# First quarter of a linear-attention kernel: alpha, key and query fetched as three-token runs, and another order of the first weight pieces

## The chip, the cores and the metric

The kernel runs on one core of one Trainium2 chip. The metric is the device time of one launch in microseconds (us), the median of three runs.

## The reference, cut to what matters

Three stages follow each other: a gated linear attention (a state of 48 by 48 for each head, decayed by alpha at each token), a SiLU-gated feed-forward layer behind an RMS norm, and a second layer with four experts that are weighted by domain probabilities.

```python
for t in range(S):                       # B=2, H=8, S=768, D=48
    state = alpha[:, :, t, :, None] * state + einsum('bhd,bhe->bhde', k[:, :, t], v[:, :, t])
    y[:, :, t] = einsum('bhd,bhde->bhe', q[:, :, t], state)
x = y.transpose(0, 2, 1, 3).reshape(1536, 384)
xn = x / sqrt(mean(x * x) + 1e-6) * rms_g
x = (silu(xn @ w_gate) * (xn @ w_val)) @ w_out          # 384 -> 1536 -> 384
out = sum over e of p[:, e] * (relu(x @ w1[e]) @ w2[e]) # 4 experts, 384 -> 1024 -> 384
```

## The kernel before, in words

The 1536 tokens are cut into four quarters of 384, a quarter into three chunks of 128. Within a quarter the eight heads are taken in four pairs. For one pair the alpha, key and query rows are transposed on TensorE (`T`, `TK`, `TQ`), VectorE makes the running product of alpha (a scan over a chunk) and scaled keys and queries (`M`), TensorE makes scores and a key-value sum (`S`, `KV`), VectorE masks the scores (`S`) and carries the state (`ST`), and TensorE adds up the output (`Y`). The first quarter's steps stand in a list written out by hand, `FIRST`; the later quarters' attention steps are placed between the matmuls of the first feed-forward layer by the generator `events()`. Every engine runs its own instructions of that one order, and semaphores tie them together.

`a_tm`, `k_tm` and `q_tm` hold a quarter token by token: partition p holds token p of each chunk, and a head takes 64 columns, 48 of data and 16 that were set to one. `load_quarter` fills them with one DMA per chunk, in rows of 48 floats (192 bytes). The first quarter is loaded in two halves of four heads; the last four heads come first, because pair 3 goes first. Alpha is clamped in place by VectorE (step `C`). All of alpha is also loaded a second time (`alpha_all`, eight parts) and tested on ScalarE for values outside the range (steps `E 0` to `E 7`).

The weights of the first layer are cut into twelve pieces, gate, val and out for each of four column groups. A piece goes into one of two staging slots (`load_piece(n)` waits in front of its DMA until piece n-2 has been split), and POOL splits it into a high and a low part: one `TENSOR_SCALAR` over 1152 elements, then three `TENSOR_TENSOR` over 384 (`split`). The semaphore `s_wlo` counts finished splits. POOL splits the first `EARLY` pieces ahead of everything else, and then one piece per step `V` of the first quarter. In step `V 0` the pieces of work on POOL are: `hidden_lo(0)`, the high part of the next piece, `hidden_lo(1)`, the low part. `hidden_lo(n)` is what TensorE needs for its matmuls of step `O n`. The first matmuls of this layer, `G 0` and `V 0`, need pieces gate 0 and val 0, `O 0` to `O 2` need out 0, `G 3` and `V 3` need gate 1 and val 1.

All loads are issued by SyncE (SP), one after another. A wait in front of one DMA holds all behind it. `fill_holes(0)` is six small DMAs of that queue: they bring the rows of the last head pair from `x_last` into the gaps of `x_raw`, and the norm, and so the first feed-forward matmul, waits for the last of them. `next_a(1)`, `next_kq(1)` and `next_v(1)` load the second quarter, three DMAs for each of alpha, key, query and value. TensorE needs its query rows in the transposes (`TQ`) just ahead of `O 0`.

```python
def load_piece(n):
    m, g = PIECES[n]
    slot = n % 2
    if n >= 2:
        sp.wait_ge(s_wlo, n - 1)
        sp.wait_ge(s_whi, n - 1)
...
if i == 0 and f < NPIECE - EARLY:
    split(pool, EARLY + f, None if f else lambda: hidden_lo(1))
```

Of the kernel before, what the change touches and what calls it, by code (L numbers as in the profile page):

```python
# [12 lines left out]
P = 128  # L13
LANE = 64
CH = 128
NCH = 3
# [10 lines left out]
def gated_attention_two_moe(nc, q, k, v, alpha, w_gate, w_val, w_out, rms_g, probs, w1, w2, out):  # L27
# [16 lines left out]
    with ctx:  # L44
        def sem(name):
            return ctx.enter_context(nc.semaphore(name))
# [81 lines left out]
        wvh = sb("wvh", [P, KT, FF], F32R, reg_b)  # L128
        wvl = sb("wvl", [P, KT, FF], F32R, reg_b)
        woh = sb("woh", [P, FT, DM], F32R, reg_b)  # L130
        reg_w = ExitStack()
# [108 lines left out]
        s_half = [sem(f"s_half{i}") for i in range(4)]  # L240
        s_clamp = sem("s_clamp")
        s_w = [sem("s_w0"), sem("s_w1")]
# [113 lines left out]
        PW = FF // NQ  # L356
        PIECES = [(m, g) for g in range(NQ) for m in ("gate", "val", "out")]
        EARLY = 3
        HI = {"gate": wgh, "val": wvh, "out": woh}
# [31 lines left out]
        for place in AT.values():  # L391
# [8 lines left out]
        FIRST = [(name, int(f)) for name, f in  # L400
                 (step.split() for step in ("F 10", "C 0", "T 0", "T 1", "TK 0", "TQ 0", "TK 1", "TQ 1", "F 5", "M 0",
# [45 lines left out]
        def _(sp):  # L447
            def load_quarter(i, which, first_head=0, last_head=H, arrived=None):
                b, t0 = i // QB, (i % QB) * TQ
                hs = slice(first_head, last_head)  # L450
                src, dst, done = ((alpha, a_tm, s_qka[0]), (k, k_tm, s_qka[1]), (q, q_tm, s_qka[2]), (v, v_tm, s_v))[which]
                for c in range(NCH):
                    sp.dma_start(dst[:, c, :].rearrange("p (h x) -> p h x", h=H)[:, hs, 0:D],  # L453
                                 src[b, hs, t0 + c * CH:t0 + (c + 1) * CH, :].rearrange("h p d -> p h d")
                                 ).then_inc(arrived or done, 16)
# [45 lines left out]
            for which in (0, 1, 2):  # L501
                load_quarter(0, which, 0, H // 2)
                if which == 0:
                    load_alphas(0)
            load_alphas(1)
            load_alphas(2)
            load_quarter(0, 3, 0, H // 2)
            load_alphas(3)
# [6 lines left out]
            rows_to_lanes(sp, gcol[:, :].rearrange("p (j n) -> p j n", n=1), rms_g.rearrange("(r n) -> r n", n=1),  # L515
                          s_small, True)
            fill_holes(0)
            next_a(1)
            load_piece(2)
            next_kq(1)  # L520
            sp.dma_start(prob[:, :, :], probs.rearrange("(t p) e -> p t e", p=P)).then_inc(s_prob, 16)
            load_piece(3)
            sp.wait_ge(s_wild, 1)
# [83 lines left out]
        def _(pool):  # L607
# [42 lines left out]
            assert made[0] == CONST_ALL  # L650

            for n in range(EARLY):
                split(pool, n)
# [105 lines left out]
        def _(act):  # L759
# [11 lines left out]
            def squares(j, done=s_sq):  # L771
                act.activation(x_nrm[:, j, :], x_raw[:, j, :], ACT.Square).then_inc(done, 1)

            for name, i, f in events():
                u = NP * i + f
# [186 lines left out]
        def _(dve):  # L962
# [59 lines left out]
            for name, i, f in events():  # L1022
                u = NP * i + f
                if name == "C":

                    part = a_tm[:, :, :]
                    if i == 0:
                        part = a_tm[:, :, 0:H // 2 * LANE] if f else a_tm[:, :, H // 2 * LANE:]
                    if i == 0 and f == 0:
                        dve.wait_ge(s_half[0], 16 * NCH)  # L1030
                    else:
                        dve.wait_ge(s_qka[0], 16 * NCH * (i + 1))
                    dve.tensor_scalar(part, part, MID - HALF, MID + HALF, ALU.max, ALU.min).then_inc(s_clamp, 1)
                elif name == "T":
# [294 lines left out]
        def _(pe):  # L1329
# [21 lines left out]
            for name, i, f in events():  # L1351
# [11 lines left out]
                if name in ("T", "TK", "TQ", "AHEAD"):  # L1363
# [3 lines left out]
                    for which, tm, bank, done in todo:  # L1367
                        if which and i == 0 and f < 2:
                            pe.wait_ge(s_half[which], 16 * NCH)
                        elif which:  # L1370
                            pe.wait_ge(s_qka[which], 16 * NCH * (i + 1))
                        else:

                            pe.wait_ge(s_clamp, 1 if i == 0 and f < 2 else i + 2)
                            if i and f == 0:
                                pe.wait_ge(s_rinv, i)
                            wait_two(pe, s_sm, i, f, 2)
                        if which == 1:
                            wait_two(pe, s_st, i, f, NCH)
                        if which == 2 and i:  # L1380
                            pe.wait_ge(s_wild, 1)
                            wait_three(pe, s_yc, i, f, 2)
                        for c in range(NCH):
                            mm = pe.transpose(banks[bank][:, c * CH:(c + 1) * CH],  # L1384
                                              tm[:, c, n * 2 * LANE:(n + 1) * 2 * LANE], ident[:, :])
                        mm.then_inc(done, 1)
# [247 lines left out]
```

## Time and profile before

| | us |
|---|---|
| median of three runs | 700.92 |
| lowest and highest | 700.06 and 701.42 |
| the profiled execution's own time | 701.39 |
| its span on the chip | 699.3 |
| TensorE busy | 685.6 |
| VectorE, ScalarE, POOL busy | 460.1, 260.1, 320.1 |

The span runs from the first to the last instruction; what lies around it is 2.1 us. TensorE is busy for 98% of the span. The times in the rows further down are counted from the span's start.

### The profile page before, as it was taken

The numbers are of one execution on the slowest core, as the hardware profiler recorded it, in microseconds if no ns is written. First come the engines' busy times: TensorE is split into PE (matmuls) and PEld (weight loads), VectorE is DVE, ScalarE is ACT, GpSimd is POOL, SyncE is SP. The second block draws the span as 40 slices with busy tenths as digits, with TensorE's granted clock in tenths as the row PEclk, the third lists the DMA queues.
The fourth block names the chain that finished last, engine by engine and source line by source line (L and its number), as shares of the span: only waits on it lengthen the run. The fifth ranks groups of instructions, "written<-read, shape, count | busy, mean of one in ns | idle before, by whom it ended". The sixth has DMA issues, their size and how long they took to land.

```text
span 699.3 us, 10687 instructions
## 1 busy us (share of the span) xinstructions
PE 685.6 (98%) x3998; PEld 635.2 (91%) x3998; DVE 460.1 (66%) x808; ACT 260.1 (37%) x472; POOL 320.1 (46%) x401
## 2 busy tenths in 40 slices
PE   7799999999999999999999999999999999999998
PEld 6689999999999999998899999999999999999997
DVE  6875666655556543306848777877797778777875
ACT  4831334222522243227314343434343334433430
POOL 3469761121111114740394585458645764577200
PEclk9999999999999999999999999999999999999999
DMA  8994480005102000100001101110011101100003
GB/s 183 207 198 112 102 171 0 9 1 103 35 1 77 1 2 27 65 0 1 1 22 47 46 5 42 46 46 22 24 46 46 38 9 46 45 24 1 23 0 136
DMA packets 71748, 35.13 MB, mean 50 GB/s; under 512 B 53904, under 2 KB 70672, under 8 KB 71696
## 3 DMA queue, kind: packets, MB, share of 16 engines
q1 hardware_dynamic: 71696, 34.44, 19.7%
q8 instruction: 32, 0.52, 0.3%
q14 instruction: 20, 0.16, 0.1%
HBM read 31.48 MB, written 2.36 MB: 48 GB/s over the span
## 4 chain that ended last, share of the span: by engine, by line
PE 89%; SPq 6%; DVE 2%; issue 1%; DMA 1%; POOL 1%; ACT 0%; DVEq 0%
PE out_ps L1341 13%; PE out_ps L1343 13%; PE out_ps L1342 13%; PE hid_ps L1334 7%; PE hid_ps L1336 7%; PE hid_ps L1335 7%; PE at_ps L1546 4%; PE at_ps L1545 4%; PE at_ps L1544 4%; SPq L453 4%; PE hid_ps L1545 2%; PE hid_ps L1546 2%; PE hid_ps L1544 2%; PE at_ps L1384 2%; SPq L444 1%; PE at_ps L1398 1%
## 5 line engine op out<-in xcount | busy, mean ns | idle before, releaser
L1216 DVE SCALAR_TENSOR_TENSOR x<-out_ps,prob,x 128x384 f32<-128x384 f32 x180 | 110.4, 613 | 58.7 <-PE out_ps L1343 58.7
L1341 PE MATMUL out_ps<-early_r,late_r 128*128 128x384 f32 x384 | 129.1, 336 | 0.3 <-DVE x L1216 0.3
L1342 PE MATMUL out_ps<-early_r,late_r 128*128 128x384 f32 x384 | 129.4, 337 | 0.0
L1343 PE MATMUL out_ps<-early_r,late_r 128*128 128x384 f32 x384 | 129.3, 337 | 0.0
L671 POOL TENSOR_TENSOR hid_lo<-act_sb,hid_hi 128x384 fp32r<-128x384 f32 x44 | 44.9, 1020 | 167.6 <-ACT hid_hi L859 167.6
L915 ACT COPY late<-at_ps 128x512 f32<-128x512 f32 x98 | 57.7, 589 | 108.0 <-PE at_ps L1546 105.1
L1181 DVE TENSOR_TENSOR act_sb<-hid_ps,act_sb 128x384 f32<-128x384 f32 x48 | 26.6, 555 | 80.2 <-PE hid_ps L1336 70.9
L1341 PEld LDWEIGHTS out_ps<-early_r,late_r 128*128 128x128 f32 x384 | 72.1, 188 | 6.6 <-DVE x L1216 0.9
L1342 PEld LDWEIGHTS out_ps<-early_r,late_r 128*128 128x128 f32 x384 | 72.0, 188 | 5.3
L1343 PEld LDWEIGHTS out_ps<-early_r,late_r 128*128 128x128 f32 x384 | 72.1, 188 | 0.0
L725 POOL TENSOR_TENSOR early<-stage 128x128 f32<-128x128 f32 x14 | 6.5, 465 | 129.6 <-PE at_ps L1546 102.6
L859 ACT CAST hid_hi<-act_sb 128x384 fp32r<-128x384 f32 x48 | 24.6, 513 | 107.9 <-DVE act_sb L1181 107.9
L1341 PE MATMUL out_ps<-hid_hi,woh 128*128 128x384 f32 x144 | 50.8, 352 | 0.6 <-DVE hid_lo L1185 0.6
L1334 PE MATMUL hid_ps<-xn_hi,wvh 128*128 128x384 f32 x141 | 49.3, 349 | 0.8 <-POOL wvl L603 0.7
L1546 PE MATMUL at_ps<-late_r,early_r 128*128 128x512 f32 x126 | 50.0, 397 | 0.0
L1334 PE MATMUL hid_ps<-xn_hi,wgh 128*128 128x384 f32 x141 | 49.2, 349 | 0.2 <-DVE act_sb L1168 0.2
L1269 DVE TENSOR_TENSOR at_ps<-at_ps,late 128x512 f32<-128x512 f32 x70 | 48.7, 695 | 0.5
L1544 PE MATMUL at_ps<-late_r,early_r 128*128 128x512 f32 x126 | 48.9, 388 | 0.0
L1343 PE MATMUL out_ps<-hid_hi,wol 128*128 128x384 f32 x144 | 48.3, 335 | 0.0
L1342 PE MATMUL out_ps<-hid_lo,woh 128*128 128x384 f32 x144 | 48.2, 335 | 0.0
L1336 PE MATMUL hid_ps<-xn_hi,wvl 128*128 128x384 f32 x141 | 47.3, 335 | 0.0
L1335 PE MATMUL hid_ps<-xn_lo,wvh 128*128 128x384 f32 x141 | 47.2, 335 | 0.0
(272 smaller groups left out, 1613.7 us busy)
## 6 DMA issues: line engine op xcount, KB each, us to landing
stage<-in_moe_w_dram SPq DMA_DIRECT2D x32, 384.0 KB, 3.4
alpha_all<-in_alpha_dram SPq DMA_DIRECT2D x8, 288.0 KB, 6.8
stage<-in_moe_w_out_dram SPq DMA_DIRECT2D x4, 576.0 KB, 4.1
out_dram<-x SPq DMA_DIRECT2D x12, 192.0 KB, 1.9
stage<-in_moe_w_gate_dram SPq DMA_DIRECT2D x8, 216.0 KB, 4.0
stage<-in_moe_w_val_dram SPq DMA_DIRECT2D x8, 216.0 KB, 4.1
a_tm<-in_alpha_dram SPq DMA_DIRECT2D x9, 192.0 KB, 4.1
k_tm<-in_k_dram SPq DMA_DIRECT2D x9, 192.0 KB, 4.4
```

The source lines that it names most:

```text
L671: pool.tensor_tensor(hid_lo[:, n % 2, :], act_sb[:, n % 2, :], hid_hi[:, n % 2, :].bitcast(F32), ALU.subtract).then_inc(s_hl, 1)
L915: act.copy(tcp[n], bank).then_inc(s_copy, 1)
L1216: dve.scalar_tensor_tensor(out=a, in0=part, scalar=p, in1=a, op0=ALU.mult, op1=ALU.add).then_inc(s_acc, 1)
L1269: dve.tensor_tensor(bank, bank, tcp[part], op).then_inc(s_add, 1)
L1334: pe.matmul(dst, ah, bh, start=(n == 0), stop=False)
L1335: pe.matmul(dst, ah, bl, start=False, stop=False)
L1336: mm = pe.matmul(dst, al, bh, start=False, stop=(n == last))
L1341: pe.matmul(dst, ah, bh, start=first, stop=False)
L1342: pe.matmul(dst, ah, bl, start=False, stop=False)
L1343: return pe.matmul(dst, al, bh, start=False, stop=last)
L1544: pe.matmul(bank, ah, bh, start=first, stop=False, skip_group_check=True)
L1546: pe.matmul(bank, al, bh, start=False, stop=True, skip_group_check=True).then_inc(s_mul, 1)
```

## The change

The alpha, key and query loads of the first quarter become one DMA per half. Each puts three tokens that follow one another onto a partition, a run of 576 bytes, in a new tile `runs`, which shares its memory with `woh`. A copy then lays `runs` out into `a_tm`, `k_tm` and `q_tm`. For the first half it is the clamp on VectorE (alpha) and two copies on ScalarE; for the second half all three are on POOL, where the alpha clamp of VectorE (`C 1`) goes as well. Since partition p now holds tokens 3p to 3p+2, the transposes write their columns with a step of three. In the queue of SP, value's second half goes ahead of `alpha_all` part 2.

The order of the pieces becomes gate 0, val 0, gate 1, out 0, val 1, out 1. `EARLY` is 4 instead of 3, and `load_piece(2)` stands ahead of `fill_holes(0)`. In `FIRST` the warm-up goes from 10 to 8 matmuls, `E 0` goes ahead of `KS 0`.

```diff
+        runs = sb("runs", [P, 3, H, NCH * D], stack=reg_r)
...
-        PIECES = [(m, g) for g in range(NQ) for m in ("gate", "val", "out")]
-        EARLY = 3
+        PIECES = [("gate", 0), ("val", 0), ("gate", 1), ("out", 0), ("val", 1), ("out", 1)]
+        PIECES += [(m, g) for g in range(2, NQ) for m in ("gate", "val", "out")]
+        EARLY = 4
+
+        def run_parts(which, first_head, last_head):
+
+            tm, hs = (a_tm, k_tm, q_tm)[which], slice(first_head, last_head)
+            return (tm[:, :, :].rearrange("p c (h x) -> p c h x", h=H)[:, :, hs, 0:D],
+                    runs[:, which, hs, :].rearrange("p h (c d) -> p c h d", c=NCH))
...
-                 (step.split() for step in ("F 10", "C 0", "T 0", "T 1", "TK 0", "TQ 0", "TK 1", "TQ 1", "F 5", "M 0",
-                                            "M 1", "S 0", "KS 0", "E 0", "C 1", "S 1", "KS 1", "T 2", "E 1", "KV 0",
+                 (step.split() for step in ("F 8", "C 0", "T 0", "T 1", "TK 0", "TQ 0", "TK 1", "TQ 1", "F 5", "M 0",
+                                            "M 1", "S 0", "E 0", "KS 0", "S 1", "KS 1", "T 2", "E 1", "KV 0",
...
+                if i == 0 and which < 3:
+                    sp.dma_start(runs[:, which, hs, :], (alpha, k, q)[which][b, hs, t0:t0 + TQ, :].rearrange(
+                        "h (p c) d -> p h (c d)", c=NCH)).then_inc(arrived or s_qka[which], 16)
+                    return
...
             load_alphas(1)
+            load_quarter(0, 3, 0, H // 2)
             load_alphas(2)
-            load_quarter(0, 3, 0, H // 2)
...
+            load_piece(2)
             fill_holes(0)
             next_a(1)
-            load_piece(2)
+            load_piece(3)
             next_kq(1)
             sp.dma_start(prob[:, :, :], probs.rearrange("(t p) e -> p t e", p=P)).then_inc(s_prob, 16)
-            load_piece(3)
...
+            a_half, a_run = run_parts(0, 0, H // 2)
+            pool.wait_ge(s_qka[0], 16)
+            pool.tensor_scalar(a_half, a_run, MID - HALF, MID + HALF, ALU.max, ALU.min).then_inc(s_clamp_b, 1)
+            for which in (1, 2):
+                half, run = run_parts(which, 0, H // 2)
+                pool.wait_ge(s_qka[which], 16)
+                pool.tensor_copy(half, run).then_inc(s_run_b[which], 1)
...
+            for which in (1, 2):
+                half, run = run_parts(which, H // 2, H)
+                act.wait_ge(s_half[which], 16)
+                act.copy(half, run).then_inc(s_run[which], 1)
...
+                            to = bass.ds(c, CH, step=NCH) if i == 0 else slice(c * CH, (c + 1) * CH)
+                            mm = pe.transpose(banks[bank][:, to],
                                               tm[:, c, n * 2 * LANE:(n + 1) * 2 * LANE], ident[:, :])
```

On SP, from the parameter `rms_g` (`gcol`) to the probabilities, the queue of before reads as follows; `stage` is a weight piece, `x_raw<-x_last` is `fill_holes(0)`, and `a_tm`, `k_tm`, `q_tm` belong to the second quarter.

```order
L444 DMA gcol<-in_moe_rms_g_dram 16x3x1
L462 DMA x_raw<-x_last 16x384 [waits s_yc]
L462 DMA x_raw<-x_last 16x384 x5
L453 DMA a_tm<-in_alpha_dram 128x8x48 [waits s_ta]
L453 DMA a_tm<-in_alpha_dram 128x8x48 x2
L473 DMA stage<-in_moe_w_out_dram 128x3x384 [waits s_whi,s_wlo]
```

The same place in the changed kernel:

```order
L458 DMA gcol<-in_moe_rms_g_dram 16x3x1
L458 DMA stage<-in_moe_w_gate_dram 48x3x384 [waits s_whi,s_wlo]
L458 DMA stage<-in_moe_w_gate_dram 16x3x384
L458 DMA stage<-in_moe_w_gate_dram 48x3x384
L458 DMA stage<-in_moe_w_gate_dram 16x3x384
L480 DMA x_raw<-x_last 16x384 [waits s_yc]
```

Four DMAs of gate 1 and their wait for the first finished split stand ahead of `fill_holes(0)` now; they stood behind the probabilities.

On POOL, behind the split of out 0, the kernel before has this order (`wgh` and `wgl` are high and low part of a gate piece):

```order
L603 TENSOR_TENSOR wol<-stage,woh 128x384
L671 TENSOR_TENSOR hid_lo<-act_sb,hid_hi 128x384 [waits s_hh]
L596 TENSOR_SCALAR wgh<-stage 128x3x384 [waits s_w1]
L671 TENSOR_TENSOR hid_lo<-act_sb,hid_hi 128x384 [waits s_hh]
L601 TENSOR_TENSOR wgl<-stage,wgh 128x384 [waits s_whi]
```

and the changed kernel this one:

```order
L621 TENSOR_TENSOR wol<-stage,woh 128x384
L697 TENSOR_TENSOR hid_lo<-act_sb,hid_hi 128x384 [waits s_hh]
L614 TENSOR_SCALAR wvh<-stage 128x3x384 [waits s_w0]
L697 TENSOR_TENSOR hid_lo<-act_sb,hid_hi 128x384 [waits s_hh]
L619 TENSOR_TENSOR wvl<-stage,wvh 128x384 [waits s_whi]
```

The second `hid_lo` is `hidden_lo(1)`. The piece whose arrival is waited for ahead of it was gate 1 and is val 1, which SP issues behind `next_v(1)`.

On ScalarE the changed kernel begins with these rows, where the kernel before has one table load and then the first `ACTIVATE`:

```order
L803 ACT_TABLE_LOAD
L803 COPY k_tm<-runs 128x3x4x48 [waits s_half1]
L803 COPY q_tm<-runs 128x3x4x48 [waits s_half2]
L819 ACT_TABLE_LOAD
L819 ACTIVATE at_ps<-dec 128x384 [waits s_dec]
```

Two copies and a second table load stand ahead of the first reciprocal root.

## Rows read from the trace of the kernel before

**Rows 1.** The page: the span, and the chain that ended last, by engine.

```profile
span 699.3 us, 10687 instructions
...
PE 89%; SPq 6%; DVE 2%; issue 1%; DMA 1%; POOL 1%; ACT 0%; DVEq 0%
```

**Rows 2.** Timeline of TensorE: start, length, instruction, idle time before it and its releaser.

```profile
44.22 0.49 PE L1384 MATMUL at_ps<-ident,q_tm 128*128 128x128 f32 x3
44.47 0.42 PE L1341 MATMUL out_ps<-hid_hi,woh 128*128 128x384 f32 x1
...
50.83 0.44 PE L1341 MATMUL out_ps<-hid_hi,woh 128*128 128x384 f32 x1
...
57.81 0.44 PE L1334 MATMUL hid_ps<-xn_hi,wvh 128*128 128x384 f32 x1 [0.68 <-POOL wvl L603]
```

**Rows 3.** Timeline of SP, DMA issues.

```profile
0.81 1.55 SPq L453 DMA_DIRECT2D a_tm<-in_alpha_dram  x3
...
9.00 0.51 SPq L496 DMA_DIRECT2D alpha_all<-in_alpha_dram  x1
...
16.70 2.89 SPq L444 DMA_DIRECT2D stage<-in_moe_w_gate_dram  x4
...
24.84 3.75 SPq L462 DMA_DIRECT2D x_raw<-x_last  x6
28.63 3.53 SPq L453 DMA_DIRECT2D a_tm<-in_alpha_dram  x3
```

**Rows 4.** Timeline of POOL.

```profile
26.19 1.15 POOL L596 TENSOR_SCALAR wgh<-stage 128x1152 fp32r<-128x1152 f32 x1 [18.21 <-DMA stage<-in_moe_w_gate_dram]
...
29.36 1.02 POOL L603 TENSOR_TENSOR wgl<-stage,wgh 128x384 fp32r<-128x384 f32 x1
...
37.95 1.16 POOL L596 TENSOR_SCALAR woh<-stage 128x1152 fp32r<-128x1152 f32 x1 [1.13 <-DVE xn_lo L1154]
...
42.88 1.01 POOL L671 TENSOR_TENSOR hid_lo<-act_sb,hid_hi 128x384 fp32r<-128x384 f32 x1
47.93 1.16 POOL L596 TENSOR_SCALAR wgh<-stage 128x1152 fp32r<-128x1152 f32 x1 [4.04 <-DMA stage<-in_moe_w_gate_dram]
49.05 1.01 POOL L671 TENSOR_TENSOR hid_lo<-act_sb,hid_hi 128x384 fp32r<-128x384 f32 x1
```

**Rows 5.** Timeline of ScalarE.

```profile
0.81 1.28 ACT L789 ACT_TABLE_LOAD   x1 [0.81 <-PEq L1623]
7.22 0.49 ACT L789 ACTIVATE at_ps<-dec 128x384 f32<-128x384 f32 x1 [5.13 <-DVE dec L1039]
...
12.31 0.78 ACT L766 ACTIVATE alpha_all<-alpha_all,consts 128x576 f32<-128x576 f32 x1 [1.22 <-DMA alpha_all<-in_alpha_dram]
...
33.76 0.94 ACT L772 ACTIVATE x_nrm<-x_raw 128x384 f32<-128x384 f32 x2 [1.50 <-DMA x_raw<-x_last]
```

**Rows 6.** Timeline of VectorE.

```profile
8.26 0.56 DVE L1061 TENSOR_TENSOR idec<-at_ps,dec 128x384 f32<-128x384 f32 x1
...
13.43 0.67 DVE L1033 TENSOR_SCALAR a_tm<-a_tm 128x768 f32<-128x768 f32 x1
...
29.80 2.31 DVE L1105 COPY x_raw<-hid_ps 48x384 f32<-48x384 f32 x4
```

**Rows 7.** DMA traffic: 5 to 10 us (192-byte packets alone), then 18 to 26 us.

```profile
DMA packets 4818, 0.90 MB, mean 179 GB/s; under 512 B 4818, under 2 KB 4818, under 8 KB 4818
...
DMA packets 1277, 2.06 MB, mean 257 GB/s; under 512 B 234, under 2 KB 704, under 8 KB 1277
```

**Rows 8.** One line's DMA issues, 161 to 171 us: the third quarter's alpha and query.

```profile
L453 SPq DMA_DIRECT2D a_tm<-in_alpha_dram x3: 374/583/780, 161.6 to 162.6; - x3
...
L453 SPq DMA_DIRECT2D q_tm<-in_q_dram x3: 706/790/1145, 167.2 to 169.2; - x3
...
DMA to landing us min/median/max: 3.0/3.6/4.5
```

**Rows 9.** DMA landing times of `fill_holes`, second quarter, 60 to 75 us.

```profile
DMA to landing us min/median/max: 2.3/2.8/3.5
```

More of the change, by code:

```diff
@@ L129, in gated_attention_two_moe @@
         wvl = sb("wvl", [P, KT, FF], F32R, reg_b)
+        reg_r = ExitStack()
+        runs = sb("runs", [P, 3, H, NCH * D], stack=reg_r)
+        reg_r.close()
+        assert 3 * H * NCH * D <= FT * DM
         woh = sb("woh", [P, FT, DM], F32R, reg_b)
@@ L240, in gated_attention_two_moe @@
         s_half = [sem(f"s_half{i}") for i in range(4)]
-        s_clamp = sem("s_clamp")
+        s_clamp, s_clamp_b = sem("s_clamp"), sem("s_clamp_b")
+        s_run = [None, sem("s_run_k"), sem("s_run_q")]
+        s_run_b = [None, sem("s_run_kb"), sem("s_run_qb")]
         s_w = [sem("s_w0"), sem("s_w1")]
@@ L1024, in _ @@
                 if name == "C":
-                    part = a_tm[:, :, :]
+                    part = run = a_tm[:, :, :]
                     if i == 0:
-                        part = a_tm[:, :, 0:H // 2 * LANE] if f else a_tm[:, :, H // 2 * LANE:]
-                    if i == 0 and f == 0:
-                        dve.wait_ge(s_half[0], 16 * NCH)
-                    else:
-                        dve.wait_ge(s_qka[0], 16 * NCH * (i + 1))
-                    dve.tensor_scalar(part, part, MID - HALF, MID + HALF, ALU.max, ALU.min).then_inc(s_clamp, 1)
+                        part, run = run_parts(0, H // 2, H)
+                        dve.wait_ge(s_half[0], 16)
+                    else:
+                        dve.wait_ge(s_qka[0], 16 + 16 * NCH * i)
+                    dve.tensor_scalar(part, run, MID - HALF, MID + HALF, ALU.max, ALU.min).then_inc(s_clamp, 1)
                 elif name == "T":
@@ L1367, in _ @@
                     for which, tm, bank, done in todo:
-                        if which and i == 0 and f < 2:
-                            pe.wait_ge(s_half[which], 16 * NCH)
+                        if which and i == 0:
+                            pe.wait_ge((s_run if f < 2 else s_run_b)[which], 1)
                         elif which:
-                            pe.wait_ge(s_qka[which], 16 * NCH * (i + 1))
+                            pe.wait_ge(s_qka[which], 16 + 16 * NCH * i)
                         else:
-                            pe.wait_ge(s_clamp, 1 if i == 0 and f < 2 else i + 2)
+                            if i == 0 and f >= 2:
+                                pe.wait_ge(s_clamp_b, 1)
+                            else:
+                                pe.wait_ge(s_clamp, i + 1)
                             if i and f == 0:
@@ L1383, in _ @@
                         for c in range(NCH):
-                            mm = pe.transpose(banks[bank][:, c * CH:(c + 1) * CH],
+                            to = bass.ds(c, CH, step=NCH) if i == 0 else slice(c * CH, (c + 1) * CH)
+                            mm = pe.transpose(banks[bank][:, to],
                                               tm[:, c, n * 2 * LANE:(n + 1) * 2 * LANE], ident[:, :])
```

## Prediction

> **What bounds the kernel now.** I read the chain that ended last first: TensorE holds 89% of it and the DMA issues of SP 6%, with nothing else above 2% [rows 1]. So time can be won or lost only where TensorE stands still, and most of that is in the first 60 us. There the timelines of SP, POOL and TensorE belong side by side. SP issues without a pause up to 28.59 us (24.84 + 3.75), a DMA about every 0.55 us (29 of them from 0.81 to 16.70) [rows 3]. The first gate piece, issued from 16.70, reaches POOL only at 26.19 [rows 3, 4]: SP runs ahead of a full transfer queue. `fill_holes` is issued from 24.84, and its last transfer lets the norm start on ScalarE at 33.76 [rows 3, 5]. From there TensorE runs almost without a gap; the reader sees one stall for a weight piece, 0.68 us before 57.81, for the split of val 1 [rows 2]. Three near misses don't show as stalls: the query transposes of the second quarter at 44.22, `O 0` at 44.47, whose `hidden_lo(0)` ended at 43.89 (42.88 + 1.01), and `O 1` at 50.83, whose `hidden_lo(1)` ended at 50.06 (49.05 + 1.01) [rows 2, 4].
>
> **The first half's loads.** Twelve DMA issues disappear (18 become 6), 6.6 us of SP's time at 0.55. The bytes stay: six halves of 0.295 MB, 1.77 MB in all. Such packets moved at 179 GB/s, 9.9 us for all; longer packets moved at 257 GB/s on average over 18 to 26 us [rows 7]. No row shows 576-byte packets. One bound is that they are no faster than the short ones (saving 0), the other that the piece moves forward with its issue (6.6). I place them near the rows of long packets: 257 to 310 GB/s gives 6.9 to 5.7 us, a saving of 3.0 to 4.2; I take 3.7. The first gate piece then lands at 26.19 - 3.7 = 22.5. Its split takes POOL 4.19 (26.19 to 30.38) [rows 4] and ends at W = 26.7.
>
> The Trainium skill, "DMA: Bandwidth & Descriptors", section Specifications, puts the line for full rate at 512 bytes, with an extra read and write back below it. Rows 7 agree in direction. By the page's rule alone the saving would be the upper end, 4.2, and the forecast 0.5 us lower.
>
> **The start on the engines.** One alpha DMA instead of three could start the clamp about 0.9 us sooner (two issues of 0.52 fewer). But ScalarE now has two copies of 576 elements (0.78 each at most, from an ACTIVATE of that width [rows 5]) and a second table load of 1.28 [rows 5] ahead of the first root. The third run is issued at about 1.9, its data is third in line at 0.95 to 1.15 us each, and it lands at 5.8 to 6.6. Copy and table load bring the root to 7.9 to 8.7, against 7.22 [rows 5]. VectorE's work from 8.26 on waits for it, and so starts 0.7 to 1.5 late; the clamp of 0.67 that goes to POOL comes back [rows 6]. VectorE's last copy of the attention ended at 32.11 (29.80 + 2.31) [rows 6] and would end at 32.1 to 33.0. This costs nothing as long as `fill_holes` lands later than that, which is next. If that cover is gone, it costs up to 0.8. POOL's three new operations run while it waits for the first piece, in its 18.21 us of idle time [rows 4]; the two warm-up matmuls fewer lie ahead of the first clamp.
>
> The Trainium skill, "ScalarE: Activation LUTs", section "What ACT_TABLE_LOAD costs", counts a drain of 1.38 us to each load, 2.66 in all. The row shows 1.28 for the load, with no work ahead of it that would have to drain. By the page VectorE would end at up to 34.4, about as `fill_holes` lands, and 0.3 us more could be lost.
>
> **`load_piece(2)` ahead of `fill_holes`.** SP reaches this place at about 18 and now waits until W, since the split of the first piece must be done. Four issues of about 0.48 follow, then six holes in 3.75 [rows 3]: the last starts at W + 5.1. In the second quarter such a transfer took 2.3 to 3.5 [rows 9]; I take 2.3, since the DMA queue has run low by then. The holes are there at W + 7.4 = 34.1, against 33.76: the first layer starts 0.3 late, though SP was given 6.6 us.
>
> **The stream behind it.** `next_a(1)` is issued from W + 5.8 = 32.5, against 28.63 [rows 3]. In the third quarter nine loads of this size took a first landing after 3.0 and 1.02 for each further one (161.6 + 3.0 to about 169.2 + 3.6, eight steps) [rows 8]. So alpha has landed at W + 10.9. Behind it stand out 0, key, query, the probabilities, value and val 1. Five of them have 0.59 MB each, which takes 2.3 (at 257 GB/s, rows 7) to 3.06 (three times 1.02); I take 2.7, and 0.8 for the probabilities. Out 0 lands at W + 13.6 = 40.3, query at W + 19.0 = 45.7, val 1 at W + 25.2 = 51.9.
>
> `O 0`: the split of out 0 started at 37.95, on the norm's account, and took 4.93 to 42.88 [rows 4]. Now it starts at 40.3, `hidden_lo(0)` is done at 46.2, and `O 0` starts 1.7 late (46.2 - 44.47). The query transposes wait in that same time.
>
> `O 1`: `hidden_lo(1)` stands behind the high part of val 1 on POOL. That part waits for a piece that SP issues behind `next_v(1)`; before, it was gate 1, there at 47.93, issued ahead of it [rows 4]. Val 1 at 51.9, plus 1.15, 0.1 and 1.0, gives 54.2, against 50.83: 3.4 late. `O 1` is where the two delays are settled; this one contains the 1.7 and the 0.3.
>
> `V 3`: its stall of 0.68 [rows 2] is gone, since val 1's low part is done about 3.0 after 54.2, at 57.2, and TensorE gets there at 57.1 + 3.4 = 60.5. `G 3` finds gate 1 long split. The sum is +3.4 - 0.7 = **+2.7 us**. Against the profiled execution's own 701.39 that is 704.1, span 702.0; this execution is 0.5 above the median, so I give 700.92 + 2.7 = **703.6**. Nothing behind gives it back, TensorE having no other gap worth naming.
>
> **The rivals.**
> *The queue follows the issue.* If the first piece lands 6.6 earlier, the split ends at W = 23.8, the holes land at 31.2, and VectorE's end near 32.5 decides: the layer starts 1.3 early. But val 1 lands at 49.0 and `O 1` starts at 51.3, 0.5 late; with the 0.68 back the sum is -0.2, 700.7. For it speaks that the first part of `alpha_all`, issued at 9.00, was there 3.3 later [rows 3, 5]; against it that the first piece took 9.5 us from its first issue [rows 3, 4].
>
> *Faster: val 1 arrives before it is missed.* The point is val 1's landing at about 48.3, from where `hidden_lo(1)` is done by 50.6. It takes W = 23.8 and a stream limited by SP's issues: 23.8 + 5.8, then 8.3 for alpha, key and query (161.6 to 169.9) [rows 8], 2.8 for the three value loads at the same pace, about 4 for out 0, the probabilities and the piece (seven issues or fewer near 0.55), and 3.0 to land is 47.7. Then the early start of 1.3 and the 0.68 both stay: -2.0, 698.9. Against it: the nine loads of the third quarter ran at the pace of their transfers in an otherwise empty queue [rows 8].
>
> *Slower still: no gain from the long runs.* With 576-byte packets no faster than 192-byte ones, W is 30.4 again, and by the same sum it is 2.7 + 3.7 = +6.4, 707.3. Rows 7 speak against it.
>
> **How the numbers follow.** This kernel's measurement can tell about 0.2%, 1.4 us, from no change. The forecast's mechanism, `hidden_lo(1)` behind a late val 1, has 0.60; the queue that follows the issue 0.22; faster 0.12; no gain from the runs 0.06. Within the forecast, W moves by 0.6 either way and five transfer steps by 0.4 each, 2.6 if all fell together, of which I take 2.0: 0.7 to 4.7 is its own range, 701.6 to 705.6, and a tenth of its chance (0.06) is under 1.4. That gives slower 0.60, same 0.28, faster 0.12. The range reaches from 700.2, which takes in the second case, to 705.9.
>
> **What would show it.** Right: an SP wait ahead of the gate DMAs that ends with POOL's first split between 26 and 27.5; `x_nrm` released by `x_raw` at about 34; TensorE idle before `O 0` for 1 to 2 us and before `O 1` for about 1.7 more, the latter released by POOL's `hid_lo`; no stall at `V 3`; two table loads ahead of the first root. Wrong: the first split done before 24, val 1 landed before 49, or `O 1` released by something other than `hid_lo`.

## The result, and the profile after

| | before | changed |
|---|---|---|
| median | 700.75 us (699.72 to 701.42, 5 runs) | 704.3 us (702.68 to 705.61, 5 runs) |
| profiled execution | 701.39 us, span 699.3 us | 705.61 us, span 703.8 us |
| mean granted clock of TensorE | 0.999 | 0.995 |

The ratio is 1.0055, with a 95% interval of 1.0035 to 1.0075: the change costs 3.6 us. The profiled execution of the changed kernel is 1.3 us above its median, so the sizes below are those of one of its longer runs.

The page of the changed kernel has the same chain as before [rows 1]: TensorE, and a few per cent of SP.

```profile
span 703.8 us, 10672 instructions
PE 90%; SPq 5%; DMA 2%; DVE 1%; POOL 1%; issue 1%; ACT 0%; DVEq 0%
```

The timeline of SP (start, length, line, what it issues) shows the first gate piece from 12.61 instead of 16.70 [rows 3], and then the wait that the prediction spoke of: the second gate piece is issued at 25.08, and the holes only behind it, 2.02 later than before [rows 3].

```profile
12.61 1.86 SPq L458 DMA_DIRECT2D stage<-in_moe_w_gate_dram  x4
...
25.08 1.74 SPq L458 DMA_DIRECT2D stage<-in_moe_w_gate_dram  x4
26.86 4.24 SPq L480 DMA_DIRECT2D x_raw<-x_last  x6
31.15 2.14 SPq L471 DMA_DIRECT2D a_tm<-in_alpha_dram  x3
...
43.40 2.60 SPq L471 DMA_DIRECT2D v_tm<-in_v_dram  x3
46.10 2.60 SPq L458 DMA_DIRECT2D stage<-in_moe_w_val_dram  x4
```

POOL's timeline answers to [rows 4]. The first piece is there at 20.86 instead of 26.19, and its split ends at 25.05 (24.04 + 1.01), where SP's wait ends. Out 0 is there at 38.16. The last three rows are the ones that cost: `hidden_lo(1)` stands behind the high part of val 1, and POOL has been idle for 8.59 us when that piece lands at 52.66.

```profile
20.86 1.15 POOL L614 TENSOR_SCALAR wgh<-stage 128x1152 fp32r<-128x1152 f32 x1 [7.89 <-DMA stage<-in_moe_w_gate_dram]
...
24.04 1.01 POOL L621 TENSOR_TENSOR wgl<-stage,wgh 128x384 fp32r<-128x384 f32 x1
...
38.16 1.16 POOL L614 TENSOR_SCALAR woh<-stage 128x1152 fp32r<-128x1152 f32 x1 [2.56 <-DMA stage<-in_moe_w_out_dram]
...
43.06 1.01 POOL L697 TENSOR_TENSOR hid_lo<-act_sb,hid_hi 128x384 fp32r<-128x384 f32 x1
52.66 1.15 POOL L614 TENSOR_SCALAR wvh<-stage 128x1152 fp32r<-128x1152 f32 x1 [8.59 <-DMA stage<-in_moe_w_val_dram]
53.77 0.99 POOL L697 TENSOR_TENSOR hid_lo<-act_sb,hid_hi 128x384 fp32r<-128x384 f32 x1
```

TensorE's timeline answers to [rows 2]. In this order the rows are the first matmul of `G 1`, the query transposes, `O 0`, `O 1`, one of `O 1`'s products with the low part of the weight, `G 3` and `V 3`:

```profile
40.33 0.41 PE L1363 MATMUL hid_ps<-xn_hi,wgh 128*128 128x384 f32 x1 [0.22 <-DVE act_sb L1197]
...
45.12 0.55 PE L1416 MATMUL at_ps<-ident,q_tm 128*128 128x128 f32 x3 [0.75 <-DMA q_tm<-in_q_dram]
45.42 0.42 PE L1370 MATMUL out_ps<-hid_hi,woh 128*128 128x384 f32 x1
...
54.81 0.44 PE L1370 MATMUL out_ps<-hid_hi,woh 128*128 128x384 f32 x1 [3.29 <-POOL hid_lo L697]
...
55.35 0.52 PE L1372 MATMUL out_ps<-hid_hi,wol 128*128 128x384 f32 x1
...
58.58 0.43 PE L1363 MATMUL hid_ps<-xn_hi,wgh 128*128 128x384 f32 x1
...
62.41 0.42 PE L1363 MATMUL hid_ps<-xn_hi,wvh 128*128 128x384 f32 x1
```

Side by side with before, the 4.5 us of the span come about like this. `G 1` starts at 40.33 in both: the first layer is not late. `O 0` is 0.95 late (44.47 to 45.42), of which 0.75 is a wait for the query. `O 1` is 3.98 late (50.83 to 54.81), and its row names the releaser, POOL's `hid_lo`. `G 3` started at 53.04 before and is 5.54 late. `V 3` is 4.60 late (57.81 to 62.41): its stall of 0.68 is gone, with no bracket behind its row. From there on the two run alike, and the ends differ by 4.5.

What happens between `O 1` and `G 3` was in no step of the prediction. `G 3` follows `O 1` by 3.77 us here (54.81 to 58.58) and by 2.21 before, where its row is this:

```profile
53.04 0.44 PE L1334 MATMUL hid_ps<-xn_hi,wgh 128*128 128x384 f32 x1
```

The table of windows (length, then PE, PEld, DVE, ACT and POOL busy with their counts, the granted clock, the DMA share and GB/s) has a clock of 0.55 in this stretch. It has 0.57 in another, from 14 to 18. TensorE had waited 1.86 us for the first roots, until 11.30, and 0.67 more until 13.31; up to 14 the clock was still 1.00. In the execution before, the granted clock is 1.00 from 14 to 18 and from 50 to 60.

```profile
54.80:58.50 3.70, 3.69 (x15) 3.67 (x15) 0.00 (x0) 0.00 (x0) 3.70 (x4) 0.55 0.02 4
14.00:18.00 4.00, 4.00 (x30) 3.78 (x28) 3.44 (x10) 1.07 (x3) 0.00 (x0) 0.57 1.04 242
```

So TensorE stood still for 3.29 us, and of the 3.7 us behind that it worked all but the first few tenths at 1.2 GHz, before it was given 2.4 GHz again. The row of 0.52 us shows the same: a matmul of this shape takes 0.33 to 0.34 in the stretches with a clock of 1.00.

The Trainium skill, "TensorE: Matmul & The Clock Gate", section "What you observe", says that matmuls run nearly twice as slowly at first and become fast in sustained work. The trace agrees for the work behind this stall, with 0.52 against 0.34.

The start on ScalarE answers to [rows 5]. The table load now stands behind a copy, at 7.08, and the first root starts at 8.38, against 7.22 before.

```profile
6.40 0.67 ACT L803 COPY q_tm<-runs 128x576 f32<-128x576 f32 x1 [0.98 <-DMA runs<-in_q_dram]
7.08 1.28 ACT L819 ACT_TABLE_LOAD   x1
8.38 0.49 ACT L819 ACTIVATE at_ps<-dec 128x384 f32<-128x384 f32 x1
...
32.90 0.92 ACT L798 ACTIVATE x_nrm<-x_raw 128x384 f32<-128x384 f32 x2
```

VectorE's timeline shows what that does at the end of the attention: the last copies end at 33.28 (30.97 + 2.31), against 32.11 before [rows 6], and VectorE's own share of the norm's squares follows at 33.60 and ends at 34.73. TensorE's norm matmul starts at 34.78.

```profile
30.97 2.31 DVE L1134 COPY x_raw<-hid_ps 48x384 f32<-48x384 f32 x4
...
33.60 1.13 DVE L1140 TENSOR_TENSOR x_nrm<-x_raw 128x384 f32<-128x384 f32 x1
```

### The profile page after: what moved, and what is told of

It is laid out like the page before. It is cut to its first block, busy times and chain, and to the rows that moved or that the text cites. A ratio compares the mean times of both kernels' runs of the same rounds, so it can differ in the third digit from the quotient of the medians.

```text
span 703.8 us, 10672 instructions
## 1 busy us (share of the span) xinstructions
PE 687.5 (98%) x3994; PEld 637.2 (91%) x3994; DVE 459.1 (65%) x807; ACT 262.2 (37%) x475; POOL 323.0 (46%) x404
## 4 chain that ended last, share of the span: by engine, by line
PE 90%; SPq 5%; DMA 2%; DVE 1%; POOL 1%; issue 1%; ACT 0%; DVEq 0%
PE out_ps L1370 13%; PE out_ps L1372 13%; PE out_ps L1371 13%; PE hid_ps L1363 7%; PE hid_ps L1365 7%; PE hid_ps L1364 7%; PE at_ps L1578 4%; PE at_ps L1577 4%; PE at_ps L1576 4%; SPq L471 2%; PE hid_ps L1577 2%; PE hid_ps L1578 2%; PE hid_ps L1576 2%; PE at_ps L1416 2%; PE at_ps L1430 1%; PE at_ps L1462 1%
```

## The experiments

The theory: SP's stream, held until the first split is done and carrying value ahead of val 1, brings val 1 late; `hidden_lo(1)` stands behind its split on POOL, and `O 1` waits. The rivals: the late start on ScalarE (the table load) carries through, or the layout of the runs on the engines costs the time, or the late holes do. Ratios are to the kernel before, in runs on the same chip, with 95% intervals. The changed kernel's own 704.3 comes from another series, so a difference from it is rougher than a ratio.

### Taking POOL's order away: `e1_hidlo_first`

```diff
-                        split(pool, EARLY + f, None if f else lambda: hidden_lo(1))
+                        if f == 0:
+                            hidden_lo(1)
+                        split(pool, EARLY + f)
```

> The changed kernel with one edit: on POOL, hidden_lo(1) goes ahead of the split of val 1 instead of into its middle. Theory A (TensorE loses its time at O 1 because hidden_lo(1) stands behind a piece that lands at 52.6): O 1 starts near 51.8 instead of 54.81, 3.0 us earlier, and the half-clock stretch behind the stall (1.6 us) goes too; V 3 is reached near 58.1, after val 1's split near 56.9. 4.6 us less than the changed kernel, 699.7, about the kernel before. Theory B (the DMA stream as a whole is late since load_piece(2) stands ahead of fill_holes, so a stall moves but does not go): the stall turns up at V 3 and at most 1.5 us come back, 702.8.

Measured: 702.03 us, ratio 1.0019 (1.0008 to 1.0031). POOL's and TensorE's timelines show that `hid_lo` no longer waits for val 1, that `O 1` starts without a wait, and that a stall opens one block later:

```profile
48.81 1.02 POOL L697 TENSOR_TENSOR hid_lo<-act_sb,hid_hi 128x384 fp32r<-128x384 f32 x1 [4.89 <-ACT hid_hi L891]
...
51.49 1.15 POOL L614 TENSOR_SCALAR wvh<-stage 128x1152 fp32r<-128x1152 f32 x1 [1.66 <-DMA stage<-in_moe_w_val_dram]
```

```profile
51.23 0.44 PE L1372 MATMUL out_ps<-hid_hi,woh 128*128 128x384 f32 x1
...
60.88 0.44 PE L1372 MATMUL out_ps<-hid_hi,woh 128*128 128x384 f32 x1 [1.46 <-POOL hid_lo L697]
```

The stall at `O 1` is gone, as theory A has it, and 2.3 us of 3.6 come back, where A expected 4.6 and B at most 1.5. The late piece itself is not cured: its split and that of out 1 now push `hidden_lo(2)`, and `O 2` waits 1.46 us. Neither theory named that place; B looked for the stall at `V 3`.

### Taking the late piece away: `e2_val1_before_value`

```diff
+            load_piece(4)
             next_v(1)
-            for n in range(4, NPIECE):
+            for n in range(5, NPIECE):
```

> The changed kernel with one edit: SP issues val 1 (load_piece(4)) ahead of next_v(1). Theory A: val 1 lands near 49.3, hidden_lo(1) is done by 51.5, O 1 starts near 51.8, value lands near 52.6 and is needed near 53.5: 4.6 us less than the changed kernel, 699.7. Theory B: value is now missed by the key-value sums of the second quarter, 1 us or more of it stays: 701 to 703.

Measured: 700.93 us, ratio 0.9996 (0.9987 to 1.0006). Val 1 lands before `hidden_lo(1)` is due, and `O 1` has no bracket:

```profile
49.35 1.15 POOL L615 TENSOR_SCALAR wvh<-stage 128x1152 fp32r<-128x1152 f32 x1 [4.01 <-DMA stage<-in_moe_w_val_dram]
50.47 1.01 POOL L698 TENSOR_TENSOR hid_lo<-act_sb,hid_hi 128x384 fp32r<-128x384 f32 x1
```

```profile
52.64 0.44 PE L1371 MATMUL out_ps<-hid_hi,woh 128*128 128x384 f32 x1
```

One piece issued ahead of three value loads gives back all that the change cost: 3.4 us, where theory A expected 4.6. Everything else of the change is still in this kernel: the runs, the copies, the second table load, the wait ahead of the holes. Taken together these cost and gain nothing, although the stall at `V 3` is gone too; what each does singly this run doesn't show.

### The two parts apart: `e3_runs_alone` and `e4_order_alone`

`e3_runs_alone` is the kernel before with the runs, their layout on three engines, and the small changes that go with them, and with the order of the pieces and of SP's queue as it was. `e4_order_alone` is the rest:

```diff
-        PIECES = [(m, g) for g in range(NQ) for m in ("gate", "val", "out")]
-        EARLY = 3
+        PIECES = [("gate", 0), ("val", 0), ("gate", 1), ("out", 0), ("val", 1), ("out", 1)]
+        PIECES += [(m, g) for g in range(2, NQ) for m in ("gate", "val", "out")]
+        EARLY = 4
...
+            load_piece(2)
             fill_holes(0)
             next_a(1)
-            load_piece(2)
+            load_piece(3)
             next_kq(1)
...
-            load_piece(3)
```

> The changed kernel with the old piece order, EARLY 3, and fill_holes ahead of all later pieces: only the run loads, the layout copies and the front of the step list are new. Theory A: the start of the first layer is at 36.5 as in both kernels, the stream behind fill_holes is 1.5 to 2 us earlier than before, no stall at V 3: 700.75 - 0.7 = 700.0. Theory B: the second table load and the later attention show in full, about 1 us: 701.8. If the norm is bound by the holes and these land near 30, the end of the attention decides.

> The kernel before with the new piece order, EARLY 4 and load_piece(2) ahead of fill_holes, without the run loads. The first split ends near 30.4, so the holes are issued from 32.3 and land near 38.3: the first layer starts 4.5 us late. Theory A: val 1 lands 27.6 after the first split as in the changed kernel, near 58, and O 1 is 9.4 late; with the half clock (1.6) and less the old stall of 0.7 the sum is +10.3, 711. Theory B (only the late start counts): +4.5, 705.3.

Measured: the runs alone 701.0 us, ratio 1.0002 (0.9992 to 1.0011); the order alone 709.46 us (4 runs), ratio 1.0119 (1.0104 to 1.0133). In the order alone the two longest stalls on TensorE are at the norm and at `O 1`. Its clock is 1.00 behind the first:

```profile
36.52 2.20 PE L1450 MATMUL at_ps<-x_nrm,ones 128*128 128x384 f32 x6 [2.87 <-DVE x_nrm L1112]
...
57.97 0.69 PE L1342 MATMUL out_ps<-hid_hi,woh 128*128 128x384 f32 x1 [3.67 <-POOL hid_lo L672]
```

```profile
36.50:40.00 3.50, 3.48 (x15) 2.69 (x16) 3.13 (x4) 2.51 (x5) 2.13 (x2) 1.00 0.99 225
```

The order costs 8.5 us by itself, the runs nothing, and both together 3.6. In the new order the runs are worth some 5 us, since SP's wait ends with the first split, which ends at 28.35 in `e4_order_alone`; in the old order the time doesn't move. What the change lost, it lost by its order. The order alone was expected at 711 by theory A, with a first split at 30.4; that split came 2.0 earlier, and the time was 1.5 less. The runs alone lie between their two theories (700.0 and 701.8).

### The half clock behind the stall: `e5_warm_in_stall`

Seven matmuls into a free bank, ahead of `O 1`'s wait, in the changed kernel; their results are used by nothing.

```diff
                     n = FT * i + f
+                    if n == 1:
+                        pe.wait_ge(s_h, 3)
+                        keep_warm(7, hid_ps[1])
                     wait_lower(pe, n)
```

> The changed kernel with seven dummy matmuls on TensorE (ones by ones, into the bank of the finished V 2) ahead of the wait of O 1, which would fill the 3.3 us of waiting there. They compute nothing that is used. If the 1.56 us that TensorE loses between O 1 and G 3 are the half clock behind an idle stretch, O 1 still starts at 54.8, its matmuls take 0.34 instead of 0.52, G 3 starts near 57.0 and the time is 1.5 less than the changed kernel's, 702.8. If the clock has no part in it: 704.3.

Measured: 702.17 us (12 runs), ratio 1.0021 (1.0012 to 1.0031), which is 2.1 us less than the changed kernel. In TensorE's timeline the seven show as one group of 14 records; the windows follow it:

```profile
51.09 1.83 PE L1377 MATMUL hid_ps<-ones 128*128 128x128 f32 x14
...
53.18 0.44 PE L1370 MATMUL out_ps<-hid_hi,woh 128*128 128x384 f32 x1 [0.26 <-POOL hid_lo L697]
...
55.38 0.42 PE L1363 MATMUL hid_ps<-xn_hi,wgh 128*128 128x384 f32 x1
```

```profile
54.80:58.50 3.70, 3.70 (x35) 3.46 (x33) 1.73 (x5) 0.52 (x1) 3.62 (x5) 1.00 0.34 81
```

`O 1` is still released by `hid_lo`, yet `G 3` follows it by 2.20 us, as before the change, and the clock is 1.00. The half clock is a cost of its own, 1.56 us in these profiles. Without the seven matmuls the wait in this profile would have been 2.1 us, shorter than 3.29, and that might be a reason of its own for the full clock. Against it, the clock fell behind a wait of 1.53 in `e11_holes_first`, below, though it did not behind one of 1.46 in `e1_hidlo_first`. The times say more: the twelve runs lie between 701.40 and 703.44, and the six of `e6_one_table` on the same chip, the changed kernel but for a tiny root and with no such matmuls, between 703.86 and 706.52. The 2.1 us are more than the 1.5 that were expected, and the rest is not accounted for. That `O 1` comes at 53.18 and not at 54.81 is not due to the edit: in this profile val 1 landed at 51.01 instead of 52.66, with the same code ahead of it.

### The start on ScalarE: `e6_one_table`, `e8_runs_table` and `e9_val1_one_table`

With a root of one column put first, the profiles show a single table load ahead of the first roots. `e6_one_table` is the changed kernel with it, `e8_runs_table` is `e3_runs_alone` with it, `e9_val1_one_table` is `e2_val1_before_value` with it.

```diff
+            act.wait_ge(s_ones, 1)
+            act.activation(spark[:, :], ones[:, 0:1], ACT.Abs_reciprocal_sqrt)
             for which in (1, 2):
                 half, run = run_parts(which, H // 2, H)
```

> The changed kernel with one tiny reciprocal-root activation ahead of ScalarE's two copies, so that the right table is loaded at the start and the second load goes. Theory A (O 1 waits for a piece whose arrival hangs on SP's queue alone): the first root starts 1.3 earlier, the attention ends 1.1 earlier, but O 1 starts at 54.8 as before it: 704.3. Rival theory (the second table load, with the TensorE wait of 1.9 us and the half clock from 14 to 18 us behind it, is a part of the loss): 1 to 2 less, 702.3 to 703.3.

> The runs-alone kernel (old piece order and queue) with the same single table load. There nothing hangs on SP's queue any more, so the end of the attention decides when the first layer starts, and the second table load is on the path: the time should fall from 701.0 by the 1.1 us of the late root and by what half clock cost ahead of the first layer (up to 3 in its profile): 698 to 699.9. If the table load is hidden, 701.0.

> The kernel with val 1 ahead of value (700.93), with the single table load. As in the run beside it, the end of the attention comes 1.1 us sooner and TensorE is not left waiting ahead of its first layer; the fill_holes landings near 33 now bound the start: 1.0 to 1.8 less, 699.1 to 699.9. If the table load is hidden there: 700.9.

Measured: 705.43 us (6 runs), ratio 1.0067 (1.0051 to 1.0084), in the changed kernel, not to be told from the changed kernel's own 1.0055; 700.02 us, ratio 0.9988 (0.9977 to 0.9998), with the runs alone; 700.59 us, ratio 1.0001 (0.9993 to 1.001), with val 1 ahead of value. The first was expected at 704.3 by theory A and came 1.1 above it, with `O 1` at 56.19 and not at 54.8. The second lies just outside its 698 to 699.9, and the third is nearer to 700.9, the time for a hidden table load, than to 699.1 to 699.9. In the changed kernel TensorE's timeline has `G 1` 1.67 earlier, at 38.66, and nothing of it left at `O 1`:

```profile
38.66 0.41 PE L1366 MATMUL hid_ps<-xn_hi,wgh 128*128 128x384 f32 x1 [0.22 <-DVE act_sb L1200]
...
42.90 0.55 PE L1419 MATMUL at_ps<-ident,k_tm 128*128 128x128 f32 x3 [2.11 <-DMA k_tm<-in_k_dram]
...
46.09 0.55 PE L1419 MATMUL at_ps<-ident,q_tm 128*128 128x128 f32 x3 [1.07 <-DMA q_tm<-in_q_dram]
...
56.19 0.69 PE L1373 MATMUL out_ps<-hid_hi,woh 128*128 128x384 f32 x1 [3.69 <-POOL hid_lo L698]
```

So the second table load did delay the start of the layer, and that was worth nothing in the changed kernel, since three transfers in a row are waited for behind it, the last of them, val 1, for `O 1`. It was there at 54.02 in this profile. The rival of the late start falls. With the runs alone the early start has a little value, 0.7 us at the medians, and the stall for a split has come back:

```profile
56.71 0.45 PE L1365 MATMUL hid_ps<-xn_hi,wvh 128*128 128x384 f32 x1 [0.56 <-POOL wvl L621]
```

In `e9_val1_one_table` the query is waited for instead:

```profile
44.59 0.55 PE L1420 MATMUL at_ps<-ident,q_tm 128*128 128x128 f32 x3 [1.33 <-DMA q_tm<-in_q_dram]
```

### The holes ahead of the piece: `e11_holes_first` and `e10_best_holes_first`

The changed kernel, and `e9_val1_one_table`, with this edit:

```diff
-            load_piece(2)
             fill_holes(0)
+            load_piece(2)
```

> The changed kernel with fill_holes(0) ahead of load_piece(2) instead of behind it. Theory A: SP no longer waits for the first split (25.05) at this place but for x_last near 23.2, so everything from next_a(1) on is issued 1 to 2 us earlier; val 1 lands that much earlier and O 1 with it, and the order on POOL still stalls it: 702.3 to 703.3. If the place of load_piece(2) has no part in the loss: 704.3. If it is the main cause: 700.7.

> All three repairs in the changed kernel: val 1 ahead of value, one table load, fill_holes(0) ahead of load_piece(2). The wait of 1.3 us for the second quarter's query, the last one left beside val 1 ahead of value, shrinks by the 1.1 us or more that SP's queue gains: 699.2 to 699.8. If the query lands no earlier, 700.6.

Measured: 702.24 us (10 runs), ratio 1.003 (1.0017 to 1.0043), and 700.71 us, ratio 1.0002 (0.9993 to 1.0011; one of its eleven executions took 958.56 us, and nothing here explains it). In the first, SP's holes go out at 23.58 and val 1 lands at 51.16, 1.5 earlier; `O 1` still waits for `hid_lo`:

```profile
53.33 0.45 PE L1370 MATMUL out_ps<-hid_hi,woh 128*128 128x384 f32 x1 [1.53 <-POOL hid_lo L697]
...
56.65 0.67 PE L1363 MATMUL hid_ps<-xn_hi,wgh 128*128 128x384 f32 x1
```

```profile
55.00:57.00 2.00, 2.00 (x10) 1.99 (x10) 0.02 (x1) 0.00 (x0) 2.00 (x3) 0.50 0.03 8
```

`G 3` follows `O 1` by 3.32 us here, at half clock, which is 1.1 more than before the change.

About 2 us come back without the late holes, and the rest stays. Since val 1 also landed at 51.0 to 51.5 in two profiles with the holes where the change has them, the profile alone doesn't say how much of this is the holes and how much is the spread of that landing. The time is at the lower end of theory A. In the second kernel nothing is won, where 699.2 to 699.8 was hoped for: `G 1` now waits 1.46 us for the activation, at 40.45, and the query transposes wait 0.76.

### The runs with val 1 ahead of value: `e12_runs_val1_first`

`e8_runs_table` with `load_piece(4)` (which in its order is val 1) ahead of `next_v(1)`.

> Runs alone with one table load (700.02), and val 1 ahead of value in SP's queue. Its profile has one weight stall left, 0.6 us at V 3 for val 1's split. Val 1 lands up to 3 us earlier; POOL then finishes its split near 53.6 + 1 and V 3 starts without a wait: 699.4. If value is missed at the key-value sum near 51.6 instead, 700 or more.

Measured: 700.57 us, ratio 0.9994 (0.9982 to 1.0006). That is the second of its two expectations. The stall at `V 3` is gone, and the value loads are waited for in its place:

```profile
52.41 0.80 PE L1443 MATMUL at_ps<-v_tm,k_sm 128*112 128x96 f32 x6 [0.53 <-DMA v_tm<-in_v_dram]
```

No version is faster than the kernel before by more than 0.2%. The fastest is `e8_runs_table`, by 0.12%, with an interval that ends just below no difference (0.9998).

## Why the prediction was right, step by step

The kernel was forecast at 703.6 us, slower, by one mechanism, `hidden_lo(1)` behind a late val 1. It took 704.3, and `e1_hidlo_first` and `e2_val1_before_value` show the mechanism: take either half of it away, and `O 1` starts without a wait. The sum came out near partly by luck, because errors of opposite sign met in it: the first split came 1.7 us earlier than forecast, the stream behind it took 2.4 longer, and 1.6 of half clock was in no term.

**The first half's loads.** The saving was put at 3.7, with bounds of 0 and 6.6. It was 5.3 in the profile of the changed kernel (26.19 to 20.86), and in `e5_warm_in_stall`, with the same code up to there, the piece was there at 19.01, which is 7.2, outside the bounds. This saving is mis-sized, though its true size is less sure than these differences look. The old loads' landing moves as well: in `e4_order_alone`, whose queue up to this piece is that of the kernel before, it was there at 24.19.

```profile
24.19 1.15 POOL L597 TENSOR_SCALAR wgh<-stage 128x1152 fp32r<-128x1152 f32 x1 [16.21 <-DMA stage<-in_moe_w_gate_dram]
```

Eleven profiles have the runs, and in them it was there between 18.83 and 20.86, the changed kernel's being the latest. The saving has two parts. SP reached the piece 4.09 earlier (16.70 to 12.61), and the piece landed 8.25 after its first issue, not 9.49. In the window from 3.2 to 5 us, where 80 of 1074 packets are short ones, 323 GB/s moved, above the 257 to 310 that I took; by that alone the six halves take 5.5 and save 4.4, so the rate is not all of it. W was therefore 25.05, and 23.20 in `e5_warm_in_stall` (22.19 + 1.01), where 26.7 was forecast. The second of these is near the W of the rival "the queue follows the issue", 23.8. "The first split done before 24" stood among the signs of being wrong, and it holds in nine of the eleven profiles. As a statement on the first piece that rival was nearer.

The Trainium skill, "DMA: Bandwidth & Descriptors", section Specifications, gives packets from 512 bytes on the full rate. The trace agrees in direction, with 323 GB/s for nearly all 576-byte packets against 179 for the short ones [rows 7]; no run here shows what the full rate is.

**The stream behind it.** This is the error of the other sign. From W to val 1 I counted 25.2; it took 27.6 (25.05 to 52.66), and 27.8 in `e5_warm_in_stall` (23.20 to 51.01). Alpha was issued at W + 6.1, 0.3 behind the forecast, so 2.1 were lost in the rest. If all of it is put on the five transfers, each took about 3.1, the upper end of my 2.3 to 3.06, not 2.7. But the sum also left out a pause of SP: between the probabilities, issued by 42.31, and value, issued from 43.40, SP tests the flag `wild` and issues nothing for 1.09 us, and the transfer engines' busy share is 0.64 and 0.71 in the two microseconds from 44 to 46, against 1.04 in the next. How the 2.1 divide between the two is not shown. With a W near the rival's, val 1 landed at 51.0, not at its 49.0, and the stall came all the same. Had the stream kept to my 25.2 behind a W of 23.2, val 1 would have been there at 48.4, by my own sum about where `hidden_lo(1)` holds nothing up. Out 0, at W + 13.1, was forecast at W + 13.6.

**The start and the norm.** The late root (8.38) lies in the forecast 7.9 to 8.7. The end of the attention, 33.28, lies 0.3 above the forecast 32.1 to 33.0. The cover that I named, the late holes, was thinner than I said: the holes came with an earlier W, and the norm matmul was released when VectorE's own squares ended. The layer started with no delay instead of 0.3; with one table load it started 1.7 earlier in these profiles. As the SP stream decides behind it, that is worth nothing, by `e6_one_table`. The 34.4 that was estimated for the end of the attention with a drain did not come. The signs "released by `x_raw` at about 34" (ScalarE's `x_nrm` starts at 32.90 with no wait) and "first split between 26 and 27.5" were wrong.

**`O 0`.** Forecast 1.7 late through `hidden_lo(0)`; it was 0.95 late, mostly through the query, whose transposes started at 45.12, where its landing was forecast at 45.7. `hidden_lo(0)` ended at 44.07 and held nothing up: the split of out 0 started at 38.16, not at 40.3. So this path was wrong, and more of the delay than forecast fell to `O 1`: a wait of 3.29 in place of about 1.7.

**`O 1` and `V 3`.** Forecast 54.2, released by `hid_lo`, and a stall of 0.68 gone at `V 3`. Measured 54.81, that releaser, and no stall. These steps hold.

**Left out.** The clock. I took TensorE's speed behind a stall as given. The stall of 3.29 us was followed by a stretch at half clock, which cost 1.56 us more, and `e5_warm_in_stall` takes it away. In the changed kernel's profiled execution it makes most of the difference between the +2.7 forecast and the +4.5 of the span: 3.98 at `O 1`, plus 1.56, less 0.94 at `V 3`. The last is the stall of 0.68, which cost more than its bracket says. The bracket counts from the end of the key transposes ahead of it (56.64 + 0.49 = 57.13), and without a stall the next matmul starts 0.25 behind their start (62.16 to 62.41 in the changed kernel); from there to 57.81 it is 0.92.

**What stays open.** Val 1 landed at 52.66, 51.01 and 54.02 in three profiles with the same queue of SP, the last of them with the tiny root, and at 51.49 in `e1_hidlo_first`. The changed kernel's runs spread over 2.9 us, those of before over 1.7. What moves these landings was not tried. Nor is it shown why the new order, once its stall is cured, gains nothing over the old one: the stall of 0.68 is gone in `e2_val1_before_value`, but its profile has a stretch at half clock between 28 and 33, and the layer starts 1.8 later in it.

## What to carry to other kernels

When an issue queue is shortened, follow it to its next wait on a semaphore: here 6.6 us of issues saved ended in a wait for a split, and everything behind that wait was dated from it. An engine that runs in order turns one late operand into a stall of work that has nothing to do with it; look at what stands behind a wait, and either move the small operation ahead (2.3 us here) or bring the late transfer forward (3.4 us). A stall of a few microseconds on TensorE can cost more than its length, 1.56 us behind one of 3.29 here, so look at the granted clock afterwards; it doesn't fall behind every stall. And before a sum is built on one landing time, ask how far that landing moves from run to run: here it was 2 us for the first piece and 3 for val 1.

## What the runs showed of the hardware

- The granted clock fell to half behind some of TensorE's waits and not behind others. At `O 1` it was 0.50 at the end of the wait or within a microsecond or so of it, for a wait of 3.29 us (changed kernel), of 3.67 (`e4_order_alone`) and of 1.53 (`e11_holes_first`). It stayed at 1.00 behind a wait of 2.87 at the norm in `e4_order_alone` and of 1.46 at `O 2` in `e1_hidlo_first`. Seven small matmuls, put into the wait at `O 1`, went with a clock of 1.00. I have no rule for this.
- A short wait was enough in some executions. In `e3_runs_alone` the clock fell between 28 and 30 us, behind a wait of 0.97 that the kernel before has too, at 27.17 and at full clock. TensorE is then busy throughout 30 to 34 us at half clock, and a group of twelve matmuls takes 1.52 us instead of 0.86. The run is 2.4 us above its kernel's median, so two profiles of one kernel may differ by more than the effect that is looked for. The windows of that kernel:

```profile
30.00:32.00 2.00, 2.00 (x16) 1.74 (x17) 1.47 (x5) 1.97 (x6) 0.00 (x0) 0.50 1.03 191
32.00:34.00 2.00, 2.00 (x14) 1.39 (x12) 1.13 (x3) 1.97 (x5) 0.00 (x0) 0.50 0.94 283
```

- A copy as ScalarE's first operation brought a second table load. It took 1.28 us, and the root started 0.02 after it: no further wait for a drain shows. With a tiny root ahead of the copies, one load is left ahead of the first roots, which start at 7.08 (`e6_one_table`) and 7.45 (`e8_runs_table`).
- The clamp of 576 elements that reads a run and writes it apart took 2.13 us on POOL in all eleven profiles that have it. On VectorE it took 1.37 in the changed kernel, where 768 elements in place took 0.67 [rows 6]. But that is not a fixed cost: in the eleven profiles it took 1.07 to 1.40, and it ended between 5.29 and 5.31 in each, whenever it started. What it ended with is not shown.
